# Attention over two heads at once: raw keys and queries are transposed instead of their split parts, in a new order of work

## The chip, the cores and the metric

The kernel runs on one core of a Trainium2 chip. The metric is the device time of one execution in microseconds; of several executions the median counts. The profile is one further execution, recorded by the hardware profiler.

## What is computed

Three stages follow each other. Only the first, attention, is touched by the change.

```python
q_pool = q.reshape(B, H, S // 2, 2, D).mean(axis=3)        # B=4, H=8, S=1152, D=64
scores = scale * np.matmul(q_pool, k.transpose(0, 1, 3, 2)) # 576 x 1152 for each head
scores = scores - np.max(scores, axis=-1, keepdims=True)
attn = np.exp(scores)
attn = attn / (np.sum(attn, axis=-1, keepdims=True) + 1e-09)
return np.matmul(attn, v).astype(np.float32)
# then: mixture of experts on 2304 rows of 512 (top-1 of 8 experts), then a gated two-layer network
```

## The kernel before

Every large product is made nearly exact from rounded parts: a number x is held as hi (x rounded to the matmul's fp32r format) and lo (x - hi). In a score, one operand is 128 rows deep: 64 rows of hi of the keys and 64 rows of lo, against queries of which the part is repeated in both halves. Two matmuls then add up all four products of parts.

Attention goes through 16 pairs of heads. For a pair there are nine query tiles of 128 rows (four of each head, and tile 8, TC, with the 64 rows that are left over of both heads) against 1152 keys, 9 chunks of 128. A tile needs: scores (two halves of 512 keys into the S banks, a ring of three, and a rest of 128 into bank R), the largest of each half (VectorE), exponentials with their sums (ScalarE), transposes of the probabilities (TensorE, f32), a split of these into p_hi (ScalarE) and p_lo (VectorE), and the products with v in bank O.

The work of a pair is written out by hand as a list of units: b0 to b8 (probabilities of the second head of the pair before), c0 to c2 (its tile 8), x (turning the outputs back and dividing), a0 to a8 (the first head of this pair), and g (groups of four chunks of keys and queries of the next pair). TensorE fills a transpose bank T (a ring of three, TR) for each unit; ScalarE and VectorE empty it. The list before, SLOTS, has 33 units in nine slots, one slot a tile; scores, maxima and exponentials of the next tile are put at the first and second place of each slot. The products of a unit come two units after its transposes (LAG = 2), and the rings p_hi and p_lo have PT = 3 buffers.

Keys and queries are prepared thus (split_kq_of, L389 to L399): for each pair, GpSimd adds the two rows of each query pair and writes hi and lo of keys and queries side by side, 36 chunks of 128 columns, in 11.8 us or so of its time; this runs two pairs ahead. TensorE transposes the 36 chunks in nine groups (L697), ScalarE copies each group into kq_t with the scale (L493), and GpSimd pads the rest of the queries with zeros (pad, c_pad). The DMA queue of SyncE (SP) loads keys, queries and values, one DMA for the keys of both heads (rows of 2304 bytes), and waits with next_kq for the split, not for TensorE.

Bodies are unrolled by kind: "first" (pair 0, only a and g units), "mid" (pairs 1 to 14, a loop of two), "last" (pair 15, no g) and "tail".

Of the kernel before, what the change touches and what calls it, by code (L numbers as in the profile page):

```python
# [12 lines left out]
P = 128  # L13
# [48 lines left out]
def attention(nc, q, k, v, w_gate, w_out_gate, w1, x_dram, xs_dram, ys_dram, shared):  # L62
# [15 lines left out]

    B, H, SK, D = k.shape
# [11 lines left out]
    NT = KC + 2 * TILES  # L91
    GROUPS = NT // 4


    HALF_SCALE = (0.5 / float(D) ** 0.5) ** 0.5
    X_TILES = [(0, 3), (3, 6), (6, 8)]
# [3 lines left out]
    PT = 3  # L100


    SCORES_AT, MAXIMA_AT, EXP_AT = (0, 1), (0, 1), (0, 0, 1)
    LAG = 2
    assert (CH, QT, REM, D, PAIRS % 2, NT % 4) == (9, 4, 64, 64, 0, 0)
# [15 lines left out]
    assert all(half.shape[1] == NT * P for half in shared.x_half)  # L121
    assert HALF_SCALE == 0.25 and len([s for slot in SLOTS for s in slot]) % TR == 0 and 2 * TILES % SR == 0
    KEEP = {"first": "ag", "mid": "abcxg", "last": "abcx", "tail": "bcx"}

    def slots(kind):
        return [[s for s in slot if s[0] in KEEP[kind]] for slot in SLOTS]

    def steps(kind):
        return [s for slot in slots(kind) for s in slot]
# [7 lines left out]
    def by_act(step):  # L137

        return step[0] == "g"

    def by_dve(step):
        return not by_act(step)
# [19 lines left out]

    def lagged(kind, j):
# [5 lines left out]
    UNIT_LAST = {"a": ("a", CH - 1), "b": ("b", CH - 1), "c": ("c", 2)}  # L169

    ctx = ExitStack()
    with ctx:
# [12 lines left out]
        q_sum = sb("q_sum", [P, TILES * D])  # L185

        split_kq = [half[:, :].bitcast(F32R) for half in shared.x_half]
        v_hl = [sb(f"v_hl{i}", [P, KC * P], F32R) for i in range(2)]
        kq_t = [sb(f"kq_t{i}", [P, NT * P], F32R) for i in range(2)]
        c_pad = [sb(f"c_pad{i}", [P, 4 * P], F32R) for i in range(2)]  # L190
# [26 lines left out]
        first_q_sums = sem("first_q_sums")  # L217
        first_parts_done = sem("first_parts_done")
        kq_split = sem("kq_split")
        v_split = sem("v_split")  # L220
        c_padded = sem("c_padded")
# [7 lines left out]
        t_free_act = sem("t_free_act")  # L229
        t_free_dve = sem("t_free_dve")  # L230
# [12 lines left out]
        KQ_DMAS, X_DMAS = 5, 3  # L243
# [7 lines left out]
        def split_views(par):  # L251

            kq = split_kq[par]
            return (raw_k[:, :].rearrange("p (c d) -> p c d", d=D),
                    raw_q[:, :].rearrange("p (t r d) -> p t r d", t=TILES, r=2),
                    q_sum[:, :].rearrange("p (t d) -> p t d", d=D),
                    kq[:, 0:KC * P].rearrange("p (c s d) -> p c s d", s=2, d=D),
                    kq[:, KC * P:(KC + TILES) * P].rearrange("p (c s d) -> p c s d", s=2, d=D),
                    kq[:, (KC + TILES) * P:NT * P].rearrange("p (c s d) -> p c s d", s=2, d=D))
# [10 lines left out]
        with nc.Block() as block:  # L270

            @block.sync
            def _(sp):
                def load_kq(p):
                    sp.dma_start(raw_k[:, :].rearrange("p (h c) -> p h c", h=2),
                                 k_rows[bass.ds(2 * p, 2)].rearrange("h p c -> p h c")).then_inc(kq_loaded, 16)
# [13 lines left out]
                def next_kq(p):  # L290

                    sp.wait_ge(kq_split, p)
                    load_kq(p)

                def next_v(p):

                    sp.wait_ge(v_split, p)
                    load_v(p)

                def store(p):  # L300


                    kind = {LAST - 1: "last", LAST: "tail"}.get(p, "mid") if isinstance(p, int) else "mid"
                    sp.wait_ge(t_free_dve, upto(p + 1, kind, by_dve, ("x", 2)))
# [10 lines left out]

                load_kq(0)
                load_v(0)
                next_kq(1)
# [11 lines left out]
                next_v(1)  # L330
                next_kq(2)
                next_kq(3)
                next_v(2)
                with sp.Fori(1, LAST - 2) as p:
                    next_kq(p + 3)
                    next_v(p + 2)
                    store(p - 1)
                next_v(LAST)
# [11 lines left out]
                for p in range(LAST - 3, LAST - 1):  # L350
                    store(p)

                sp.wait_ge(t_filled, before(LAST, "last", every))
# [5 lines left out]
                store(LAST - 1)  # L359
                store(LAST)  # L360

            @block.gpsimd
            def _(pool):
                nc.gpsimd.memset(zeros[:, :], 0.0).then_inc(zeros_ready, 1)
                nc.gpsimd.memset(ident[:, :], 0.0)
                for i in range(2):
                    nc.gpsimd.memset(c_pad[i][:, :].bitcast(F32), 0.0)
# [3 lines left out]
                                        base=0, pattern=[[-1, P]], channel_multiplier=1)  # L371
                nc.gpsimd.affine_select(out=stack2[:, :], in_=stack2[:, :], compare_op=ALU.not_equal, fill=1.0,
                                        base=0, pattern=[[-1, D]], channel_multiplier=1).then_inc(pool_chain, 1)
                pool.wait_ge(pool_chain, 2)
# [10 lines left out]
                def split_kq_of(p, par, chain):  # L385

                    rk, rq, qs, kp, qh, ql = split_views(par)
                    pool.wait_ge(kq_loaded, 16 * KQ_DMAS * (p + 1))
                    nc.gpsimd.tensor_tensor(qs, rq[:, :, 0, :], rq[:, :, 1, :], ALU.add)  # L389
                    first_part(kp[:, :, 0, :], rk).then_inc(pool_chain, 1)  # L390

                    pool.wait_ge(pool_chain, chain + 1)
                    nc.gpsimd.tensor_tensor(kp[:, :, 1, :], rk, kp[:, :, 0, :].bitcast(F32), ALU.subtract)
                    first_part(qh[:, :, 0, :], qs)
                    first_part(qh[:, :, 1, :], qs).then_inc(pool_chain, 1)

                    pool.wait_ge(pool_chain, chain + 2)
                    for s in range(2):
                        last = nc.gpsimd.tensor_tensor(ql[:, :, s, :], qs, qh[:, :, 0, :].bitcast(F32), ALU.subtract)  # L399
                    last.then_inc(kq_split, 1)  # L400
# [12 lines left out]
                def pad(p, par):  # L413

                    for part in range(2):
                        for h in range(2):
                            src = (KC + part * TILES + TC) * P + h * REM
                            dst = (part * 2 + h) * P + h * REM
                            last = first_part(c_pad[par][:, dst:dst + REM], kq_t[par][:, src:src + REM].bitcast(F32))
                    last.then_inc(c_padded, 1)  # L420


                split_v_of(0, 0, 2)

                pool.wait_ge(t_free_act, before(0, "first", by_act))
                pad(0, 0)

                def body(p, par, kind):
                    chain = 3 + 3 * p
                    if kind == "first" or (kind == "mid" and not isinstance(p, int)):  # L430

                        pool.wait_ge(t_filled, before(p, kind, every))
                        split_kq_of(p + 2, par, chain)
                    else:
                        chain -= 2
# [3 lines left out]
                    split_v_of(p + 1, 1 - par, chain + 2)  # L439

                    pool.wait_ge(t_free_act, upto(p, kind, by_act, ("g", 8)))
                    pad(p + 1, 1 - par)
# [5 lines left out]

                p = LAST - 2
                pool.wait_ge(t_filled, before(p, "mid", every))  # L450
                split_kq_of(p + 2, 1, 3 + 3 * p)
                pool.wait_ge(pv_done, upto(p, "mid", is_prob, ("c", 2)))
                split_v_of(p + 1, 0, 5 + 3 * p)
                pool.wait_ge(t_free_act, upto(p, "mid", by_act, ("g", 8)))
                pad(p + 1, 0)
                body(LAST - 1, 0, "mid")

# [32 lines left out]
            def _(act):  # L490
                def group(par, g, bank):

                    nc.scalar.activation(kq_t[par][:, g * 512:g * 512 + 512], T[bank][:, :], ACT.Copy,  # L493
                                         scale=HALF_SCALE).then_inc(t_free_act, 1)
# [1362 lines left out]
```

## Time and profile before

| | us |
|---|---|
| median of 3 runs | 1524.81 |
| lowest, highest | 1521.59, 1526.77 |
| profiled execution, its time | 1529.89 |
| its span, first to last instruction | 1527.9 |
| TensorE busy (matmuls) | 1425.5 (93%) |
| VectorE busy | 854.6 (56%) |
| ScalarE busy | 684.4 (45%) |
| GpSimd busy | 504.6 (33%) |

The span is what the instructions take; the profiled execution's own time is 2 us more. Attention ends at about 657 us of the span. The shares of busy time are over all three stages: in the first one TensorE, VectorE and ScalarE are all far busier than in the others, and the table of 40 slices shows the DMA rate flat at 54 GB/s over most of attention.

### The profile page before, as it was taken

To read this page: it belongs to the slowest core of one execution; us is meant where nothing else is said; L and a number is where in the kernel's file an instruction comes from. 1 tells how busy PE (TensorE), PEld (TensorE's weight loads), DVE (VectorE), ACT (ScalarE), POOL (GpSimd) and SP (SyncE) were. 2 spreads that over 40 slices of the span, in tenths; PEclk is the share of its full clock that TensorE was granted. 3 is DMA by queue.
4 is the path that set the end of the run, shared out by engine and by line. 5 is a ranking of instruction groups with operands and counts; after the bars stand their busy time and mean duration, and the time that the engine had idled before them with its cause. 6 is when DMAs were issued, how large, how long until landed. Compare 5 with 4: busy or idle time off the path is not lost. (4 is left out here: it accounts for less than half of the span.)

```text
span 1527.9 us, 25839 instructions
## 1 busy us (share of the span) xinstructions
PE 1425.5 (93%) x8085; PEld 1236.9 (81%) x8086; DVE 854.6 (56%) x1602; ACT 684.4 (45%) x1635; POOL 504.6 (33%) x340
## 2 busy tenths in 40 slices
PE   4999999999999999983997899998999999999998
PEld 3788888888888888762786787886999999999997
DVE  4788777777777778755443444443643232323222
ACT  4878888888888887751214301101521111111111
POOL 2664444444444432047728802203201010110000
PEclk9999999999999999995998999999999999999999
DMA  7421111111111121245626713112521010100000
GB/s 263 127 56 54 54 54 54 54 54 54 54 54 54 54 65 31 75 139 206 221 96 208 245 41 96 55 41 88 157 65 35 7 35 7 34 7 21 0 21 21
DMA packets 87034, 117.00 MB, mean 77 GB/s; under 512 B 8784, under 2 KB 47696, under 8 KB 86992
## 3 DMA queue, kind: packets, MB, share of 16 engines
q1 hardware_dynamic: 71072, 74.50, 15.6%
q10 hardware_dynamic: 12880, 31.99, 6.2%
q0 software_dynamic: 3040, 9.96, 2.0%
q8 instruction: 25, 0.41, 0.1%
q14 instruction: 17, 0.14, 0.0%
HBM read 87.33 MB, written 29.10 MB: 76 GB/s over the span
## 5 line engine op out<-in xcount | busy, mean ns | idle before, releaser
L648 DVE TENSOR_TENSOR p_lo<-ps_t,p_hi 128x512 fp32r<-128x512 f32 (+1 forms) x336 | 221.3, 670 | 81.7 <-ACT p_hi L509 78.5
L509 ACT ACTIVATE p_hi<-ps_t 128x512 fp32r<-128x512 f32 (+1 forms) x336 | 193.0, 585 | 73.8 <-PE ps_t L697 71.8
L573 DVE TENSOR_REDUCE maxima<-ps_s 128x1 f32<-128x512 f32 x288 | 196.6, 683 | 33.0 <-PE ps_s L804 30.8
L1039 POOL TENSOR_TENSOR w_parts<-raw_w,w_parts 128x1024 fp32r<-128x1024 f32 x64 | 150.9, 2394 | 190.4 <-ACT w_parts L1109 190.2
L533 ACT ACTIVATE probs<-ps_s,neg_max 128x512 f32<-128x512 f32 x288 | 199.9, 694 | 15.7 <-DVE neg_max L586 15.6
L697 PE MATMUL ps_t<-ident,probs 128*128 128x128 f32 x1296 | 191.5, 273 | 0.0
L697 PEld LDWEIGHTS ps_t<-ident,probs 128*128 128x128 f32 x1296 | 156.6, 140 | 33.2
L1655 ACT ACTIVATE silu<-ps_g 128x384 f32<-128x384 f32 x72 | 35.4, 491 | 314.8 <-PE ps_g L1761 314.8
L804 PE MATMUL ps_s<-kq_t 128*128 128x512 f32 x512 | 168.1, 410 | 4.9 <-ACT probs L533 3.1
L1109 ACT ACTIVATE w_parts<-raw_w 128x1024 fp32r<-128x1024 f32 x64 | 67.0, 1057 | 222.0 <-PE ps_h L1436 105.0
L1708 DVE TENSOR_TENSOR silu<-ps_g,silu 128x384 f32<-128x384 f32 x72 | 40.1, 557 | 210.3 <-ACT silu L1655 210.2
L773 PE MATMUL ps_o<-p_hi,v_hl 128*128 128x512 f32 x288 | 138.9, 482 | 12.6 <-DVE p_lo L648 8.1
L804 PEld LDWEIGHTS ps_s<-kq_t 128*128 128x128 f32 x512 | 89.4, 189 | 30.3 <-ACT probs L533 13.5
L773 PE MATMUL ps_o<-p_lo,v_hl 128*128 128x512 f32 x288 | 113.5, 394 | 0.0
L493 ACT ACTIVATE kq_t<-ps_t 128x512 fp32r<-128x512 f32 x144 | 85.0, 604 | 44.9 <-PE ps_t L697 43.8
L1759 PE MATMUL ps_g<-mxt_hi,wg 128*128 128x384 f32 x288 | 97.6, 339 | 2.5 <-DVE mxt_lo L1683 2.4
L1617 POOL DMA_INDIRECT kept_rows<-y_by_slot,slot_i x15 | 15.7, 1048 | 250.2 <-PE ps_turn L1745 235.8
L1761 PE MATMUL ps_g<-mxt_hi,wg 128*128 128x384 f32 x288 | 97.7, 339 | 0.0
L1760 PE MATMUL ps_g<-mxt_lo,wg 128*128 128x384 f32 x288 | 97.3, 338 | 0.0
L1434 PE MATMUL ps_h<-w_parts,xst_hi 128*128 x200 | 83.2, 416 | 14.3 <-POOL w_parts L1039 12.2
L1759 PE MATMUL ps_v<-mxt_hi,wv 128*128 128x384 f32 x288 | 96.4, 335 | 0.0
L1760 PE MATMUL ps_v<-mxt_lo,wv 128*128 128x384 f32 x288 | 96.4, 335 | 0.0
(212 smaller groups left out, 3210.8 us busy)
## 6 DMA issues: line engine op xcount, KB each, us to landing
raw_w<-in_moe_w ACTq DMA_DIRECT2D x61, 512.0 KB, 4.1
raw_k<-in_k SPq DMA_DIRECT2D x16, 576.0 KB, 4.0
raw_v<-in_v SPq DMA_DIRECT2D x16, 576.0 KB, 3.8
raw_q<-in_q SPq DMA_DIRECT2D x32, 256.0 KB, 4.0
x_by_slot<-zeros SPq DMA_DIRECT2D x1, 6400.0 KB, 19.5
y_by_slot<-x_out SPq DMA_DIRECT2D x25, 256.0 KB, 2.0
kept_rows<-x_by_slot SPq DMA_DIRECT2D x23, 256.0 KB, 2.7
out<-kept_rows SPq DMA_DIRECT2D x18, 256.0 KB, 2.2
```

The lines of the kernel that those rows point to most:

```text
L493: nc.scalar.activation(kq_t[par][:, g * 512:g * 512 + 512], T[bank][:, :], ACT.Copy, scale=HALF_SCALE).then_inc(t_free_act, 1)
L509: nc.scalar.activation(p_hi[m % PT][:, 0:w], T[ring(kind, j)][:, 0:w], ACT.Copy).then_inc(hi_ready, 1)
L533: nc.scalar.activation(probs[:, at:at + 512], S[(2 * tile + h) % SR][:, :], ACT.Exp, bias=neg_max[:, tile:tile + 1], accum_out=sums[par][: ...
L573: nc.vector.reduce_max(maxima[:, 3 * tile + h:3 * tile + h + 1], S[(2 * tile + h) % SR][:, :], AX).then_inc(max_done, 1)
L648: nc.vector.tensor_tensor(p_lo[m % PT][:, 0:w], t[:, 0:w], p_hi[m % PT][:, 0:w].bitcast(F32), ALU.subtract).then_inc(t_free_dve, 1)
L697: last = nc.tensor.transpose(dst[:, n * P:(n + 1) * P], src, ident[:, :])
L773: last = nc.tensor.matmul(O[:, :], v_hl[v_par][:, c * P:(c + 1) * P], part[:, :], start=(i == 0 and n == 0), stop=(i == CH - 1 and n == 1))
L804: last = nc.tensor.matmul(S[(2 * tile + h) % SR][:, :], w, kq_t[par][:, at:at + 512], start=(n == 0), stop=(n == len(ops) - 1))
L1039: nc.gpsimd.tensor_tensor(w_part(n, parity, 1, at, PIECE), raw[j % RAW][:, :], w_part(n, parity, 0, at, PIECE).bitcast(F32), ALU.subtract) ...
L1759: nc.tensor.matmul(dst, wh, xh, start=(c == 0), stop=False)
L1760: nc.tensor.matmul(dst, wh, xl, start=False, stop=False)
L1761: last = nc.tensor.matmul(dst, wl, xh, start=False, stop=(c == DC - 1))
```

## The change

Keys and queries are no longer split before they are transposed. The raw keys of the two heads are loaded side by side (chunk, head, 64 columns), the sums of queries likewise, and 14 chunks of 128 columns (9 of keys, 5 of queries) are transposed in four groups. A transposed chunk then holds head 0 in rows 0 to 63 and head 1 in rows 64 to 127. ScalarE writes hi from the bank (group_hi), VectorE writes lo from the bank and hi (group_lo, one or two instructions), both into one tile, parts. Scores need hi and lo of one head below each other, so six DMAs (copy_parts) copy rows of parts into kq_t: for each head 64 rows of 2432 columns (hi of keys, hi and lo of queries), 64 rows of 1152 (lo of keys) and 64 rows of 1280 (queries again).

Also changed: GpSimd only adds queries (q_sums) and splits v; pad and c_pad are gone, since the zeros of q_sum give the padding. The keys come with two DMAs a pair, in runs of 64 numbers. One semaphore t_free takes the place of two. LAG is 3 and PT is 7. The list UNITS has 27 units (four g, two x), and the places of scores, maxima and exponentials are written as the number of a unit for each tile. In the SP queue next_pair waits for the last group of the pair, then issues the six copies, then the loads of the keys and queries after that, then waits for the split of v and loads v. TensorE waits ahead of g0 for the loads and the sums.

```diff
-    NT = KC + 2 * TILES
-    GROUPS = NT // 4
+    QC = QT + 1
+    KQ = CH + QC
+    HEAD = (CH + 2 * QC) * P
+    LO_Q, LO_K = KQ * P, (KQ + QC) * P
+    GROUP_CHUNKS = [(0, 4), (4, 8), (8, 12), (12, 14)]
+    GROUPS = len(GROUP_CHUNKS)
...
-    PT = 3
-    SCORES_AT, MAXIMA_AT, EXP_AT = (0, 1), (0, 1), (0, 0, 1)
-    LAG = 2
-    SLOTS = [
-        [("b", 0), ("g", 0), ("b", 1), ("g", 1)],
-        [("b", 2), ("b", 3), ("b", 4)],
-        [("b", 5), ("b", 6), ("b", 7), ("b", 8), ("g", 2)],
-        [("c", 0), ("c", 1), ("g", 3), ("c", 2), ("g", 4)],
-        [("x", 0), ("a", 0), ("a", 1)],
-        [("x", 1), ("a", 2), ("g", 5), ("g", 6), ("a", 3)],
-        [("a", 4), ("g", 7)],
-        [("g", 8), ("a", 5), ("a", 6)],
-        [("x", 2), ("a", 7), ("a", 8)],
-    ]
+    PT = 7
+    LAG = 3
+    UNITS = [
+        ("g", 0), ("b", 0), ("b", 1), ("b", 2), ("b", 3), ("b", 4), ("b", 5), ("b", 6), ("b", 7),
+        ("b", 8), ("c", 0), ("c", 1), ("c", 2), ("g", 1), ("x", 0), ("a", 0), ("x", 1), ("a", 1),
+        ("a", 2), ("g", 2), ("g", 3), ("a", 3), ("a", 4), ("a", 5), ("a", 6), ("a", 7), ("a", 8),
+    ]
+    SCORES_AT = [(25, 26), (0, 1), (2, 3), (6, 7), (10, 12), (12, 14), (16, 16), (19, 20), (22, 23)]
+    MAXIMA_AT = [(24, 25), (0, 0), (3, 3), (5, 7), (11, 12), (13, 14), (16, 16), (18, 19), (20, 22)]
+    EXP_AT = [(0, 0, 1), (2, 3, 4), (5, 5, 7), (9, 11, 12), (13, 13, 13), (16, 16, 16), (18, 19, 20), (21, 21, 22), (24, 25, 25)]
...
 load_kq(p), SP
-                    sp.dma_start(raw_k[:, :].rearrange("p (h c) -> p h c", h=2),
-                                 k_rows[bass.ds(2 * p, 2)].rearrange("h p c -> p h c")).then_inc(kq_loaded, 16)
+                    for h in range(2):
+                        sp.dma_start(raw_k[:, :].rearrange("p (c h d) -> p c h d", h=2, d=D)[:, :, h, :],
+                                     k_rows[bass.ds(2 * p + h, 1)].rearrange("h p (c d) -> (h p) c d", d=D)
+                                     ).then_inc(kq_loaded, 16)
...
+                def copy_parts(par):
+                    for h in range(2):
+                        src, at = parts[h * D:h * D + D].bitcast(F32), h * HEAD
+                        sp.dma_start(kq_t[par][0:D, at:at + HEAD].bitcast(F32), src[:, 0:LO_K]).then_inc(kq_copied, 16)
+                        sp.dma_start(kq_t[par][D:P, at:at + CH * P].bitcast(F32), src[:, LO_K:LO_K + CH * P]
+                                     ).then_inc(kq_copied, 16)
+                        sp.dma_start(kq_t[par][D:P, at + CH * P:at + HEAD].bitcast(F32), src[:, CH * P:LO_K]
+                                     ).then_inc(kq_copied, 16)
...
+                def next_pair(p, par, kind, load=True):
+                    sp.wait_ge(t_free, upto(p, kind, every, LAST_G))
+                    copy_parts(1 - par)
+                    if load:
+                        load_kq(p + 2)
+                        sp.wait_ge(v_split, p + 2)
+                        load_v(p + 2)
...
+                def q_sums(p):
+                    rq = raw_q[:, :].rearrange("p (t r d) -> p t r d", t=TILES, r=2)
                     pool.wait_ge(kq_loaded, 16 * KQ_DMAS * (p + 1))
+                    for h in range(2):
+                        tiles = slice(h * QT, (h + 1) * QT)
+                        last = nc.gpsimd.tensor_tensor(
+                            q_sum[:, 0:2 * QT * D].rearrange("p (t h d) -> p t h d", h=2, d=D)[:, :, h, :],
+                            rq[:, tiles, 0, :], rq[:, tiles, 1, :], ALU.add)
+                    last.then_inc(q_tiles_summed, 1)
+                    pool.wait_ge(q_tiles_summed, p + 1)
+                    for h in range(2):
+                        rows = slice(h * REM, (h + 1) * REM)
+                        nc.gpsimd.tensor_tensor(q_sum[rows, (2 * QT + h) * D:(2 * QT + h + 1) * D],
+                                                rq[rows, TC, 0, :], rq[rows, TC, 1, :], ALU.add).then_inc(q_summed, 1)
+                        pool.wait_ge(q_summed, 2 * p + h + 1)
...
 body(p, par, kind), GpSimd
+                    split_v_of(p + 1, 1 - par, 3 + p)
+                    if sums:
+                        pool.wait_ge(t_filled, upto(p, kind, every, LAST_G))
+                        q_sums(p + 2)
...
+                def group_lo(g, bank):
+                    c0, c1 = GROUP_CHUNKS[g]
+                    cuts = [c0] + [c for c in (CH,) if c0 < c < c1] + [c1]
+                    for a, b in zip(cuts, cuts[1:]):
+                        at = low_part(a)
+                        last = nc.vector.scalar_tensor_tensor(
+                            out=parts[:, at:at + (b - a) * P], in0=T[bank][:, (a - c0) * P:(b - c0) * P],
+                            scalar=HALF_SCALE, in1=parts[:, a * P:b * P].bitcast(F32), op0=ALU.mult,
+                            op1=ALU.subtract)
+                    last.then_inc(t_free, 1)
...
 fill of a g unit, TensorE
-                        pe.wait_ge(kq_split, p + 2)
-                        last = group(1 - par, i, t)
+                        if i == 0:
+                            pe.wait_ge(kq_loaded, 16 * KQ_DMAS * (p + 2))
+                            pe.wait_ge(q_summed, 2 * (p + 2))
+                        last = group(i, t)
...
 scores(p, par, tile, h), TensorE
-                    if tile == TC and h == 0:
-                        pe.wait_ge(c_padded, p + 1)
+                    if tile == 0 and h == 0:
+                        pe.wait_ge(kq_copied, 16 * COPIES * (p + 1))
```

## Rows read from the trace of the kernel before

**Rows 1.** Busy time by engine in one pair's period: PE, PEld, DVE, ACT, POOL.
```profile
139.40:178.30 38.90, 38.04 (x249) 32.22 (x248) 30.91 (x64) 31.44 (x84) 18.75 (x13) 1.00 0.19 53
```
**Rows 2.** Timeline of GpSimd: start, length, operation; both start a pair's body.
```profile
139.42 1.42 POOL L389 TENSOR_TENSOR q_sum<-raw_q 128x576 f32<-128x576 f32 x1 [5.96 <-PE ps_t L697]
...
489.58 1.43 POOL L389 TENSOR_TENSOR q_sum<-raw_q 128x576 f32<-128x576 f32 x1 [5.96 <-PE ps_t L697]
```
**Rows 3.** Waits in the same period: who, for whom, total, times, longest.
```profile
DVE p_lo L648 <- ACT p_hi L509: 5.2, 10, 1.3
```
**Rows 4.** Timeline of TensorE in that period: starts give the pace.
```profile
163.56 0.62 PE L804 MATMUL ps_s<-kq_t 128*128 128x512 f32 x2
164.02 0.60 PE L697 MATMUL ps_t<-ident,probs 128*128 128x128 f32 x4
164.37 0.48 PE L773 MATMUL ps_o<-p_hi,v_hl 128*128 128x512 f32 x1
...
164.92 0.63 PE L804 MATMUL ps_s<-kq_t 128*128 128x512 f32 x2
165.39 1.03 PE L697 MATMUL ps_t<-ident,kept_rows 128*128 128x128 f32 x8
166.18 0.47 PE L773 MATMUL ps_o<-p_hi,v_hl 128*128 128x512 f32 x1
...
170.75 1.20 PE L804 MATMUL ps_s<-kq_t,c_pad 128*128 128x512 f32 x4
171.78 0.60 PE L697 MATMUL ps_t<-ident,probs 128*128 128x128 f32 x4
...
176.75 1.00 PE L817 MATMUL ps_r<-kq_t 128*128 128x128 f32 x8
177.59 1.06 PE L697 MATMUL ps_t<-ident,probs 128*128 128x128 f32 x8
```
**Rows 5.** Instructions by form in that period, VectorE, then ScalarE.
```profile
L573 DVE TENSOR_REDUCE maxima<-ps_s 128x1 f32<-128x512 f32 x18 | 12.3, 683 | 1.2 <-PE ps_s L804 1.1
L648 DVE TENSOR_TENSOR p_lo<-ps_t,p_hi 128x512 fp32r<-128x512 f32 x18 | 12.2, 690 | 4.0 <-ACT p_hi L509 3.9
L648 DVE TENSOR_TENSOR p_lo<-ps_t,p_hi 128x384 fp32r<-128x384 f32 x3 | 1.7, 555 | 1.3 <-ACT p_hi L509 1.3
...
L493 ACT ACTIVATE kq_t<-ps_t 128x512 fp32r<-128x512 f32 x9 | 5.3, 604 | 2.3 <-PE ps_t L697 2.2
```
**Rows 6.** Timeline of the SP queue: issues of one pair's loads.
```profile
191.01 0.40 SPq L275 DMA_DIRECT2D raw_k<-in_k  x1
191.51 0.42 SPq L279 DMA_DIRECT2D raw_q<-in_q  x1
...
193.47 0.52 SPq L282 DMA_DIRECT2D raw_q<-in_q  x1
```
**Rows 7.** Stretches with transfers: last two columns are DMA share and GB/s.
```profile
24.00:26.00 2.00, 0.68 (x7) 0.53 (x5) 1.95 (x5) 0.00 (x0) 0.00 (x0) 1.00 1.05 408
...
192.00:193.00 1.00, 1.00 (x7) 0.78 (x7) 0.48 (x3) 0.79 (x2) 0.00 (x0) 1.00 0.91 180
...
195.00:196.00 1.00, 1.00 (x10) 1.00 (x10) 1.00 (x2) 0.50 (x1) 0.00 (x0) 1.00 1.12 269
```
**Rows 8.** DMA issues: count, KB each, median us to landing.
```profile
raw_k<-in_k SPq DMA_DIRECT2D x16, 576.0 KB, 4.0
```
**Rows 9.** Timeline of GpSimd: the padding, four instructions of 64 columns.
```profile
171.26 1.15 POOL L383 TENSOR_TENSOR c_pad<-kq_t,zeros 128x64 fp32r<-128x64 f32 x4 [5.62 <-ACT kq_t L493]
```
**Rows 10.** Timeline of TensorE at the start: first scores, first g of body 0.
```profile
22.64 1.19 PE L804 MATMUL ps_s<-kq_t 128*128 128x512 f32 x4 [0.81 <-ACT kq_t L493]
...
29.16 1.09 PE L697 MATMUL ps_t<-ident,x_half 128*128 128x128 f32 x4 [4.48 <-DVE x_half L683]
```
**Rows 11.** Stretches at the start: third column from the end is PEclk.
```profile
26.00:28.00 2.00, 0.00 (x0) 0.00 (x0) 1.94 (x3) 1.26 (x2) 0.00 (x0) 0.65 1.04 406
28.00:30.00 2.00, 0.84 (x5) 0.87 (x5) 1.01 (x2) 0.00 (x0) 0.00 (x0) 0.50 1.05 408
```

More of the change, by code:

```diff
@@ L169, in attention @@
     UNIT_LAST = {"a": ("a", CH - 1), "b": ("b", CH - 1), "c": ("c", 2)}
+    LAST_X = ("x", len(X_TILES) - 1)
+    LAST_G = ("g", GROUPS - 1)
+    assert sum(map(is_prob, UNITS)) % PT == 0 and LAG < PT
+    assert UNITS[-LAG:] == [("a", CH - LAG + j) for j in range(LAG)]
     ctx = ExitStack()
@@ L184, in attention @@
         raw_q = sb("raw_q", [P, TILES * 2 * D])
[L185 to L187 removed]
+        q_sum = sb("q_sum", [P, 2 * QC * D])
+        parts = shared.x_half[0][:, 0:LO_K + CH * P].bitcast(F32R)
         v_hl = [sb(f"v_hl{i}", [P, KC * P], F32R) for i in range(2)]
[L189 to L190 removed]
+        kq_t = [sb(f"kq_t{i}", [P, 2 * HEAD], F32R) for i in range(2)]
         probs = sb("probs", [P, TILES * SK])
@@ L411, in split_v_of, with body @@
                                             ).then_inc(v_split, 1)
[L413 to L420, printed above, removed]
-                split_v_of(0, 0, 2)
[L425 to L435, printed above, removed]
+                q_sums(0)
+                split_v_of(0, 0, 2)
+                pool.wait_ge(t_filled, GROUPS)
+                q_sums(1)
+                def body(p, par, kind, sums=True):
                     if kind != "first":
                         pool.wait_ge(pv_done, upto(p, kind, is_prob, ("c", 2)))
-                    split_v_of(p + 1, 1 - par, chain + 2)
-                    pool.wait_ge(t_free_act, upto(p, kind, by_act, ("g", 8)))
-                    pad(p + 1, 1 - par)
+                    split_v_of(p + 1, 1 - par, 3 + p)
+                    if sums:
+                        pool.wait_ge(t_filled, upto(p, kind, every, LAST_G))
+                        q_sums(p + 2)
                 body(0, 0, "first")
@@ L447, in _ @@
                     body(p + 1, 0, "mid")
[L449 to L456, printed above, removed]
+                body(LAST - 2, 1, "mid")
+                body(LAST - 1, 0, "mid", sums=False)
                 nc.gpsimd.memset(shared.ones[:, :], 1.0)
@@ L686, in _ @@
-                second_parts(0)
+                    for n, step in enumerate(UNITS):
+                        if step in steps(kind):
+                            take(p, par, kind, j, step)
+                            if lagged(kind, j) in UNIT_LAST.values():
+                                outputs(p, kind, lagged(kind, j)[0])
+                            j += 1
+                        for tile in (*range(1, TILES), 0):
+                            if kind == "tail" or (kind == "last" and tile == 0):
+                                continue
+                            of = p if tile else p + 1
+                            if MAXIMA_AT[tile][0] == n:
+                                largest_half(of, tile, 0)
+                            if MAXIMA_AT[tile][1] == n:
+                                largest_half(of, tile, 1)
+                                largest_rest(of, tile)
@@ L687, in _ @@
+                    if kind == "tail":
+                        for n in range(j, j + LAG):
+                            if lagged(kind, n) in UNIT_LAST.values():
+                                outputs(p, kind, lagged(kind, n)[0])
+                for g in range(GROUPS):
+                    dve.wait_ge(kq_hi_done, g + 1)
+                    group_lo(g, g % TR)
                 largest_half(0, 0, 0)
@@ L806, in scores, with scores_rem @@
                     last.then_inc(s_ready, 1)
-                def scores_rem(p, par, tile, waits=True):
-                    if waits:
+                def scores_rem(p, par, tile, opening=False):
+                    if not (opening and tile == 0):
                         pe.wait_ge(exp_rem_done, TILES * p + tile)
@@ L847, in _ @@
-                pe.wait_ge(consts_ready, 1)
-                pe.wait_ge(kq_split, 1)
+                    for n, step in enumerate(UNITS):
+                        if step in steps(kind):
+                            fill(p, par, kind, j, step)
+                            done = lagged(kind, j)
+                            if done is not None and is_prob(done):
+                                products(p, par, kind, j - LAG, done)
+                            j += 1
+                        for tile in (*range(1, TILES), 0):
+                            if kind == "tail" or (kind == "last" and tile == 0):
+                                continue
+                            of = (p, par) if tile else (p + 1, 1 - par)
+                            opening = kind == "first" and tile > 0
+                            if SCORES_AT[tile][0] == n:
+                                scores(*of, tile, 0, opening)
+                            if SCORES_AT[tile][1] == n:
+                                scores(*of, tile, 1, opening)
+                                if tile % QT == 0:
+                                    scores_rem(*of, tile, opening)
@@ L849, in _ @@
+                    if kind == "tail":
+                        for n in range(j, j + LAG):
+                            if is_prob(lagged(kind, n)):
+                                products(p, par, kind, n - LAG, lagged(kind, n))
+                pe.wait_ge(consts_ready, 2)
+                pe.wait_ge(kq_loaded, 16 * KQ_DMAS)
+                pe.wait_ge(q_summed, 2)
                 for g in range(GROUPS):
                     if g >= TR:
-                        pe.wait_ge(t_free_act, g - TR + 1)
@@ L853, in _ @@
-                    group(0, g, T[g % TR]).then_inc(t_filled, 1)
-                pe.wait_ge(t_free_act, before(0, "first", by_act))
-                scores(0, 0, 0, 0, waits=False)
-                scores(0, 0, 0, 1, waits=False)
-                scores_rem(0, 0, 0, waits=False)
+                        pe.wait_ge(t_free, g - TR + 1)
+                    group(g, T[g % TR]).then_inc(t_filled, 1)
+                scores(0, 0, 0, 0, True)
+                scores(0, 0, 0, 1, True)
+                scores_rem(0, 0, 0, True)
```

262 lines of the change are left out of this document (88 added, 174 removed).

## The prediction

> **What bounds the kernel now.** I read the table of 40 slices first (attention is the first 17), then the busy time of one period, the waits in it, the timelines, and last the DMA views. A pair's body takes (489.58 - 139.42) / 9 = 38.9 us [rows 2]. In it TensorE is busy for 38.0 us, VectorE 30.9, ScalarE 31.4, GpSimd 18.8, the DMA engines 19% [rows 1]. So TensorE is the bound of attention, and VectorE and ScalarE have 8 us each to spare. VectorE waits 5.2 us for ScalarE's p_hi [rows 3], which costs nothing while TensorE is full. Nothing waits for a transfer in a period: loads are issued two pairs ahead. Here the reader should see that the change touches not only TensorE's sum but this distance.
>
> **The parts that save.** TensorE: eight transposes take 166.18 - 165.39 = 0.79 us [rows 4], 0.10 each; 22 fewer (36 to 14) save 2.2 us a pair. With one x unit fewer and its last 0.9 us of idle time partly gone, TensorE's own period would be about 36.0 us. ScalarE loses nine copies of 0.60 us and gains three of that and a half one [rows 5]: 31.4 - 3.3 = 28.1. VectorE gains five instructions. The nearest row for 512 columns is p_lo at 0.69 us and for 384 at 0.555 [rows 5]; by these 0.69 + 0.69 + (0.28 + 0.56) + 0.42 = 2.6 us, so 33.5. If the new form cost as little as a maximum (0.68) nothing changes; at twice its price VectorE would be at 36 and equal to TensorE. GpSimd loses over 10 us of 18.8, all of it hidden already. LAG 3 and PT 7 take waits of TensorE for p_lo away, at most the 0.9 us above; the ring T of three still makes a fill wait for the unit three back. If nothing else happened, a period would be 36 to 37.5 us.
>
> **The chain that is added.** Raw keys, q_sum and parts exist once. TensorE may turn g0 of a body only when the loads for it have landed, and SP issues these only after VectorE's lo of g3 in the body before and after the six copies. g3 is unit 20 of 27, g0 is unit 0. So each period holds, one after the other: the work from g0 to the lo of g3 (call it W), and the chain from there back to the next g0 (call it C). The period is W + C if that is over 38.9.
>
> C, step by step. SP wakes and issues: 0.2. From an issue to the first bytes 1.0: the load issued at 191.01 [rows 6] shows no share before 192, then 0.91 [rows 7]. The copies: 2 heads x 64 rows x 4864 columns x 4 bytes = 2.49 MB. No row shows a copy from SBUF to SBUF, nor one whose ends are 64 partitions. Ends: 408 GB/s, the fastest stretch, a write of long rows from all partitions, gives 6.1 us; the slowest stretch with busy engines, 180 GB/s at a share of 0.91, so 198, gives 12.6 us [rows 7]. Every fast row has all 128 partitions at its SBUF end, and here both ends have half of them, so I take the slow end, 12.6, and keep both for the range. Then the loads, behind the copies in the same queue: keys and queries 1.18 MB in short packets, 269 GB/s [rows 7], 4.4 us (3.3 at the best neighbouring rate, 6.0 at 198). To the receipt 1.3 (an issue lands in 4.0 [rows 8], of which 1.0 is the start and about 1.6 the bytes of 576 KB). GpSimd's q_sums: 1.42 us for 576 columns [rows 2], so 0.63 for each of two of 256, and two of 64 columns at 0.3 [rows 9], with handshakes 2.2, and 0.2 for TensorE to wake: 2.4. C = 0.2 + 1.0 + 12.6 + 4.4 + 1.3 + 2.4 = 21.9 us. SP's twelve issues, about 0.6 apart [rows 6], take 7 us and lie beside the transfers.
>
> The Trainium skill has a rule that speaks against this change ("SBUF — State Buffer", section "Door 1: The DMA port swizzle (why `[64,N]` ≈ `[32,N]`)"): partitions 0 to 63 reach half of the DMA ports, so a transfer to 64 partitions is no faster than one to 32; it gives about 196 to 218 GB/s. By it the copies would take 11.4 to 12.7 us. No run here shows it yet.
>
> W, step by step. TensorE's work after the fill of g3 up to the next g0: five products at 0.55 (the two g units have none), six fills at 0.35 to 0.40, scores of tile 7's second half 0.46, of tile 8 2 x 1.03 and its rest 0.4, of tile 0 2 x 0.46 and its rests 0.84 [rows 4]: 9.7 to 10 us. TensorE needs 35.4 us a pair without idle time, so 25.3 from g0 to the fill of g3, and 1.3 more until VectorE has emptied it. VectorE's own work in that stretch: 12 b and c units 7.9, three a units 2.1, maxima of seven tiles 14 x 0.683 + 1.8, outputs, normalisers and x units 3.9, groups 2.6: 27.9 as a sum of durations, 25.3 at the ratio of union to sum of rows 1 and its forms (30.9 to 34.1). It starts with an empty pipeline: ScalarE must copy g0 before the exponential of tile 0, on which tile 1's second half waits; that is 2.5 us. W = 28 (26.5 to 29).
>
> Period = 28 + 21.9 = 49.9 us, 11.0 more than before.
>
> **The sum.** From body 1 to body 15 there are 14 periods: 154 us. The start: before, the first scores are at 22.6 and g0 of body 0 at 29.2 [rows 10]; body 1 starts at 139.42 - 2 x 38.9 = 61.6. After, loads land at 7.3 and sums at 9.5, four groups are empty at about 14, so g0 of body 0 is at 14 + 21.9 = 36, its g3 at about 58 (body 0 has only the 13 a and g units and is bound by exponentials) and g0 of body 1 at 80: 18 us later. Body 15 has no g0 and waits for the copies alone: 4 us less. 154 + 18 - 4 = 168. The profiled execution's own 1529.9 + 168 = 1698; its median of runs is 5 lower: 1693. The later stages are the same instructions; the loads of x wait for copies that are long done.
>
> What I leave out and keep in the range: TensorE stops twice a period, for the copies ahead of tile 0's scores and again ahead of g0, some 10 us in all. After 4.5 us of idle [rows 10] the granted clock is 0.65, then 0.50, that is 1.2 instead of 2.4 GHz [rows 11].
>
> **The rivals.**
> Copies at full rate: 6.1 us as by the 408 GB/s row. C = 15.4, period 43.4, 14 x 4.5 = 63, start 6, end -2: +67, 1592. For it: the engines hold that rate for 15 us at the start. Against it: half of the partitions at both ends.
> The clock too: in each period TensorE works for 3 us or more at half speed after the stops and that lies in W. +3 a pair over the forecast: 1735. For it: rows 11. Against it: the stop is in two parts, with 3 us of scores between, and VectorE sets much of W.
> The chain is hidden, and the change is faster: the DMA engines pass over the copies and serve the loads beside them, and TensorE runs ahead enough. It decides where W + C is below 38.9, with C below 10.9 at W = 28. Then the period is TensorE's and VectorE's 36 to 36.5: 15 x -2.5 = -38, 1487. Against it: with transfers that take no time, the last of twelve issues still starts at 6.6, lands 4.0 later and the sums take 2.4: C = 13.2. That would give 41 us, and 1560.
> VectorE as the bound at twice the price for the lo parts would add 2.6 to W, as part of the forecast's own range.
>
> **How the numbers follow.** Forecast (slow copies, clock little) 0.55, its own range 1660 to 1725; full-rate copies 0.27; clock too 0.12; hidden 0.06. Within the cases: faster by over 0.3% has 0.05, within 0.3% 0.01, slower 0.94; 0.3% (5 us) is about what a measurement of this kernel can tell from none. The range 1585 to 1750 holds the full-rate case, the forecast and the clock case, and leaves out the hidden one and the tails.
>
> **What would show it.** After: the period 50 us (43 to 52), with TensorE waiting ahead of L804 of tile 0 for copies into kq_t, and ahead of a transposing group for GpSimd's q_sum or the loads, 8 us or more in sum a pair; kq_t copies landing 12 to 14 us after their first issue; transposes of keys and queries 14 a pair; VectorE busy 33 to 34 us a period; DMA share up to about 0.6 of the period. It would be wrong if the copies land within 8 us, or if no wait stands ahead of g0; the step at fault would then be the copies' rate or the order of the queue.

## The result: 13% slower, and where the time went

The changed kernel takes 1722.31 us in the median of 4 runs (1717.25 to 1724.0), the kernel before 1525.79 (1521.59 to 1527.8). The ratio is 1.129, with a 95% interval of 1.125 to 1.132. 1693 was forecast, in a range of 1585 to 1750. The profiled execution has a span of 1720.3 us, 192.4 more than before.

One period of a pair, by engine (columns as in [rows 1]), then the starts of GpSimd's split of v, which comes once a body; the first of these is body 1, the last body 14:

```profile
321.10:372.20 51.10, 38.37 (x226) 32.36 (x225) 32.66 (x67) 28.89 (x80) 7.35 (x6) 0.87 0.41 89
```
```profile
111.09 2.66 POOL L397 TENSOR_TENSOR v_hl<-raw_v,zeros 128x1152 fp32r<-128x1152 f32 x1 [23.95 <-PE ps_o L762]
...
774.05 2.66 POOL L397 TENSOR_TENSOR v_hl<-raw_v,zeros 128x1152 fp32r<-128x1152 f32 x1 [22.75 <-issue]
```

The period is (774.05 - 111.09) / 13 = 51.0 us, where it was 38.9 [rows 2]; from one g0 to the next it is 51.1. TensorE's busy time has hardly changed (38.4, was 38.0 [rows 1]), though it has 22 transposes fewer: it works part of the time at half its clock (0.87 in the mean). VectorE has 32.7 instead of 30.9, ScalarE 28.9 instead of 31.4, GpSimd 7.4 instead of 18.8. The period has grown by 12 us in which TensorE stands still. The timeline of TensorE has both stops; the rows are the last g group of one pair, the first scores of the next pair, its g0, and its last g group:

```profile
318.10 0.44 PE L686 MATMUL ps_t<-ident,q_sum 128*128 128x128 f32 x2 [0.31 <-DVE p_lo L649]
...
335.19 1.19 PE L784 MATMUL ps_s<-kq_t 128*128 128x512 f32 x2 [9.86 <-DMA kq_t<-kept_rows]
...
342.32 1.12 PE L686 MATMUL ps_t<-ident,raw_k 128*128 128x128 f32 x4 [2.49 <-POOL q_sum L413]
...
369.26 0.44 PE L686 MATMUL ps_t<-ident,q_sum 128*128 128x128 f32 x2 [0.31 <-DVE p_lo L649]
```

The reader should see 9.86 us of idle time whose releaser is a copy into kq_t (the profile calls the tile parts "kept_rows"), and 2.49 us whose releaser is GpSimd's sum of queries. Neither releaser is in the waits of before. The queue of SP shows the beginning of the chain, and GpSimd's timeline its end:

```profile
321.09 0.49 SPq L295 DMA_DIRECT2D kq_t<-kept_rows  x1
321.62 0.60 SPq L296 DMA_DIRECT2D kq_t<-kept_rows  x1
322.26 2.39 SPq L298 DMA_DIRECT2D kq_t<-kept_rows  x1
...
330.61 3.46 SPq L275 DMA_DIRECT2D raw_k<-in_k  x2
...
372.25 0.50 SPq L295 DMA_DIRECT2D kq_t<-kept_rows  x1
```
```profile
340.07 1.41 POOL L405 TENSOR_TENSOR q_sum<-raw_q 128x256 f32<-128x256 f32 x2 [20.79 <-DMA raw_q<-in_q]
341.56 0.71 POOL L413 TENSOR_TENSOR q_sum<-raw_q 64x64 f32<-64x64 f32 x2
```

So C, from the first copy's issue to g0, is 342.32 - 321.09 = 21.2 us, and W, from g0 to the next first issue, 372.25 - 342.32 = 29.9. They add up to the period.

### The profile page after: what moved, and what is told of

It is laid out like the page before. It is cut to its first block and busy times, and to the rows that moved or that the text cites. A ratio compares the mean times of both kernels' runs of the same rounds, so it can differ in the third digit from the quotient of the medians.

```text
span 1720.3 us, 24853 instructions
## 1 busy us (share of the span) xinstructions
PE 1433.4 (83%) x7733; PEld 1236.4 (72%) x7734; DVE 871.5 (51%) x1658; ACT 639.0 (37%) x1549; POOL 345.1 (20%) x241
## 5 line engine op out<-in xcount | busy, mean ns | idle before, releaser
L784 PE MATMUL ps_s<-kq_t 128*128 128x512 f32 x640 | 228.7, 455 | 171.0 <-DMA kq_t<-kept_rows 163.9
L784 PEld LDWEIGHTS ps_s<-kq_t 128*128 128x128 f32 x640 | 124.9, 214 | 207.5 <-issue 154.4
L649 DVE TENSOR_TENSOR p_lo<-ps_t,p_hi 128x512 fp32r<-128x512 f32 (+1 forms) x336 | 215.0, 666 | 14.0 <-ACT p_hi L506 9.3
L686 PE MATMUL ps_t<-ident,probs 128*128 128x128 f32 x1296 | 207.5, 286 | 0.0
L686 PEld LDWEIGHTS ps_t<-ident,probs 128*128 128x128 f32 x1296 | 171.8, 149 | 46.6 <-issue 6.3
L753 PE MATMUL ps_o<-p_hi,v_hl 128*128 128x512 f32 x288 | 148.1, 514 | 1.9 <-DVE o_sb L590 1.9
L753 PE MATMUL ps_o<-p_lo,v_hl 128*128 128x512 f32 x288 | 121.0, 420 | 0.0
L397 POOL TENSOR_TENSOR v_hl<-raw_v,zeros 128x1152 fp32r<-128x1152 f32 x16 | 42.4, 2651 | 318.8 <-PE ps_o L762 295.6
L1738 PE MATMUL ps_v<-mxt_hi,wv 128*128 128x384 f32 x288 | 96.4, 335 | 0.0
L1740 PE MATMUL ps_v<-mxt_hi,wv 128*128 128x384 f32 x288 | 96.4, 335 | 0.0
```

The costliest lines, as they stand in the source:

```text
L649: nc.vector.tensor_tensor(p_lo[n][:, 0:w], t[:, 0:w], p_hi[n][:, 0:w].bitcast(F32), ALU.subtract).then_inc(t_free, 1)
L686: last = nc.tensor.transpose(dst[:, n * P:(n + 1) * P], src, ident[:, :])
L753: last = nc.tensor.matmul(O[:, :], v_hl[v_par][:, c * P:(c + 1) * P], part[:, :], start=(i == 0 and n == 0), stop=(i == CH - 1 and n == 1))
L784: last = nc.tensor.matmul(S[(2 * tile + h) % SR][:, :], w, kq_t[par][:, at:at + 512], start=(n == 0), stop=(n == len(ops) - 1))
L1738: nc.tensor.matmul(dst, wh, xh, start=(c == 0), stop=False)
L1740: last = nc.tensor.matmul(dst, wl, xh, start=False, stop=(c == DC - 1))
```

## The experiments

The ratios are against the kernel before on the same chip; chips differ by up to 0.3%, so a difference of a few us between two rows is read from their ratios. The periods are means over bodies 3 to 14, from the starts of GpSimd's split of v; the first bodies are still settling and are left out. The kernels down to LAG 2 are edits of the changed kernel; those with early groups build on one another; the last is an edit of the kernel before.

| kernel | median us | ratio, 95% interval | period us |
|---|---|---|---|
| changed kernel | 1722.31 | 1.129, 1.125 to 1.132 | 51.1 |
| copies over 128 partitions | 1639.35 | 1.075, 1.072 to 1.077 | 46.0 |
| short copies | 1622.22 | 1.062, 1.060 to 1.065 | 44.3 |
| loads ahead of copies | 1741.09 | 1.140, 1.138 to 1.142 | 52.8 |
| TensorE warm in the first stop | 1726.76 | 1.129, 1.126 to 1.132 | 51.1 |
| warm in both stops | 1703.65 | 1.115, 1.112 to 1.117 | 49.5 |
| LAG 2 | 1767.29 | 1.158, 1.155 to 1.162 | 54.2 |
| early groups | 1548.61 | 1.014, 1.012 to 1.016 | 39.1 |
| early groups, LAG 2 | 1592.16 | 1.041, 1.039 to 1.043 | 42.0 |
| early groups, zeros later | 1547.43 | 1.011, 1.009 to 1.014 | 39.1 |
| the same, x later | 1554.59 | 1.015, 1.013 to 1.017 | 39.7 |
| the same, O copied by ScalarE | 1515.82 | 0.991, 0.989 to 0.994 | 37.2 |
| kernel before, LAG 3 | 1560.04 | 1.020, 1.017 to 1.022 | 40.7 |

**Are the copies slow because of their 64 partitions?**

```diff
-                        src, at = parts[h * D:h * D + D].bitcast(F32), h * HEAD
-                        (three DMAs of 64 rows: HEAD, CH * P and HEAD - CH * P columns)
+                        at, src = h * HEAD, parts[:, :].bitcast(F32)
+                        for w0, w1 in ((0, 1216), (1216, 1792), (1792, 2432)):
+                            sp.dma_start(kq_t[par][:, at + w0:at + w1].bitcast(F32), src[:, w0:w1]
+                                         ).then_inc(kq_copied, 16)
```

> The six copies of a pair move the same 2.49 MB in six DMAs of the same bytes, but over all 128 partitions at both ends (half as many columns each). kq_t then holds the wrong rows. Theory (the copies are slow because each end reaches only half of the partitions): the copies take 6 to 7 us instead of 13, the stop ahead of tile 0's scores shrinks from 9.9 to about 3 us, the period falls from 51.1 to about 44, the kernel to about 1610 us. Rival (a copy from SBUF to SBUF runs at about 190 GB/s whatever its rows): nothing moves, 1722.

The copies now take about 6.5 us of transfer, from 338 to 344.4, and the wait for them falls to 4.47. First two stretches of the changed kernel while it copies, then two of this one (last columns: clock, DMA share, GB/s), then this one's stop:

```profile
326.00:327.00 1.00, 0.00 (x0) 0.00 (x0) 0.00 (x0) 0.97 (x4) 0.00 (x0) 1.00 1.02 214
...
332.00:333.00 1.00, 0.00 (x0) 0.00 (x0) 0.00 (x0) 0.00 (x0) 0.00 (x0) 0.50 1.04 219
```
```profile
340.00:341.00 1.00, 1.00 (x9) 0.81 (x7) 0.96 (x4) 0.87 (x2) 0.00 (x0) 1.00 1.03 397
341.00:342.00 1.00, 0.39 (x2) 0.00 (x0) 0.93 (x2) 1.00 (x4) 0.00 (x0) 1.00 1.05 421
```
```profile
345.85 1.19 PE L782 MATMUL ps_s<-kq_t 128*128 128x512 f32 x2 [4.47 <-DMA kq_t<-kept_rows]
```

At the same share of the DMA engines, the same bytes move at twice the rate. That settles the copies' price: the number of partitions, not the SBUF to SBUF path. (The edit also keeps each row at its own partition, where four of the six copies of the changed kernel move rows across to the other 64. That isn't what cost: by the bytes moved until then, the stretch from 326 lies in such copies and the one from 332 in those that keep their rows in place, and their rates are 214 and 219 GB/s.) It is also what the Trainium skill says ("SBUF — State Buffer", section "Door 1: The DMA port swizzle (why `[64,N]` ≈ `[32,N]`)"): by that rule 64 partitions move at about half; here it was 2.49 MB in 13 us (322 to 335), 192 GB/s, so the trace agrees. The bytes took 6.5 us less, but C fell only by 5.3, to 15.9 us (353.04 - 337.12), as the loads behind the copies took 6.2 us to their landing instead of 5.0. W is 29.7 and 30.7 us in turn, and the period 45.6 and 46.6, 46.0 in the mean. The expectation of 44 missed that.

**What is left without the bytes of the copies?**

```diff
-                    copy_parts(1 - par)
+                    copy_parts(1 - par, full=kind == "first")
+ (each copy of the later pairs: a, b, c = (P, P, P) columns)
```

> From the third pair on, each of the six copies moves only 128 columns (0.2 MB in all), so kq_t keeps old values elsewhere; waits and issues stay. Theory (the period is W + C, and C has the copies' bytes in it): C falls from 21.2 to about 13, bound by twelve issues, a landing and the sums; the period falls to 40 to 41 us, the kernel to about 1570. Rival (VectorE or the new order of work is what lengthens the period): it stays at 46 us or more, 1650 or above.

C is 353.59 - 339.94 = 13.7 us, near the 13.2 that the prediction had as its floor. But the period is 44.3, not 40 to 41: neither theory's number. W is 384.35 - 353.59 = 30.8 us, 0.9 more than in the changed kernel. What lengthened it is the clock: TensorE still stops for 5.62 us ahead of g0, and works at half its clock for 5 us after it, where it was 3.3 us in the changed kernel:

```profile
353.59 1.11 PE L687 MATMUL ps_t<-ident,raw_k 128*128 128x128 f32 x4 [5.62 <-POOL q_sum L414]
```
```profile
353.00:356.00 3.00, 2.41 (x8) 2.12 (x9) 0.55 (x1) 1.18 (x4) 0.46 (x2) 0.50 0.19 55
356.00:359.00 3.00, 3.00 (x11) 2.30 (x11) 0.83 (x2) 1.70 (x6) 0.00 (x0) 0.53 0.00 0
```

**Is the queue served in order?**

```diff
-                    copy_parts(1 - par)
                     if load:
                         load_kq(p + 2)
+                    copy_parts(1 - par)
```

> SP issues the loads of keys and queries ahead of the six copies. Theory (one queue, served in order, and both waits count): the loads land within 7 us and g0 no longer waits for them, but the copies land at about 19 instead of 14 us, and g0 stands behind the scores of tile 0 that wait for them; C becomes 23 to 24, the period 53 to 54, the kernel 1750 to 1760. Rival (only the loads, which come last, count, since the copies could have been hidden): the period falls to 47, the kernel to 1665.

The period is 53.2 and 52.2 in turn, 52.8 in the mean, where the theory had 53 to 54; the kernel, at 1741, is somewhat better than its 1750. The stop ahead of the scores is 15.36 us now, and there is none ahead of g0:

```profile
345.64 1.19 PE L784 MATMUL ps_s<-kq_t 128*128 128x512 f32 x2 [15.36 <-DMA kq_t<-kept_rows]
350.79 0.81 PE L686 MATMUL ps_t<-ident,raw_k 128*128 128x128 f32 x4
```

So what stands first in the queue lands first, and both of its parts are on the chain. The rival in which the loads pass by the copies falls.

**What does the clock cost?** Two kernels, the second with both edits (neither for the first pair):

```diff
 scores(...), ahead of the wait for kq_copied
+                            for n in range(85):
+                                nc.tensor.transpose(S[(2 * tile + h) % SR][:, 0:P], ident[:, :], ident[:, :])
 fill(...), ahead of the wait for kq_loaded at g0
+                                for n in range(32):
+                                    nc.tensor.transpose(t[:, 0:P], ident[:, :], ident[:, :])
```

> The changed kernel, and TensorE transposes the identity 85 times (about 9 us) into the S bank that it is about to fill, ahead of each pair's wait for the copies; nothing else moves. Theory (the stops cost more than their own length, since TensorE then works at 0.5 of its clock in W): the granted clock stays at 1.00, the work from g0 to g3 falls by 1.5 to 2.3 us, the period from 51.1 to 49 to 49.6, the kernel to about 1697. Rival (VectorE sets W, the clock costs nothing): 1722 as before, or more.

Missed: 1726.76, period 51.1. The first stop was filled, but the second grew to 4.27 us, as the scores in front of it were done sooner, and the clock fell there instead. The stretch at g0 of this kernel, then one of the kernel with both stops filled:

```profile
344.00:346.00 2.00, 1.93 (x7) 1.74 (x8) 0.07 (x1) 0.70 (x2) 0.01 (x1) 0.52 0.12 34
```
```profile
337.00:341.00 4.00, 4.00 (x24) 3.27 (x24) 2.40 (x5) 3.37 (x10) 0.00 (x0) 1.00 0.05 13
```

> As the kernel that transposes the identity 85 times ahead of the wait for the copies, and 32 times more (3.4 us) ahead of the wait of g0, into the T bank that g0 fills. In the run before this one the clock held 1.00 through the first stop and fell after the second, and the period did not move. Theory (the clock that falls after the second stop is what lengthens W): the granted clock is 1.00 at g0, the period falls from 51.1 to 49 to 49.8, the kernel to about 1700. Rival (VectorE sets W): 1722 or more.

1703.65 us, period 49.5, as expected. From g0 to the last group TensorE now takes 25.4 us instead of 26.9:

```profile
336.86 0.66 PE L686 MATMUL ps_t<-ident,raw_k 128*128 128x128 f32 x4 [0.76 <-POOL q_sum L413]
...
362.21 0.44 PE L686 MATMUL ps_t<-ident,q_sum 128*128 128x128 f32 x2 [0.31 <-DVE p_lo L649]
```

The clock thus costs 1.6 us a pair, beside the stops themselves: 19 us in the medians, 23 against the kernel before on each one's chip. Over the kernels, TensorE takes 25.4 us from g0 to the last group with no stretch at half clock behind g0, 26.9 with 3.3 us of it, and 27.8 with 5 us.

**Is it where the groups stand?** Only the list changes:

```diff
-        ("g", 0), ("b", 0), ("b", 1), ("b", 2), ("b", 3), ("b", 4), ("b", 5), ("b", 6), ("b", 7),
-        ("b", 8), ("c", 0), ("c", 1), ("c", 2), ("g", 1), ("x", 0), ("a", 0), ("x", 1), ("a", 1),
-        ("a", 2), ("g", 2), ("g", 3), ("a", 3), ("a", 4), ("a", 5), ("a", 6), ("a", 7), ("a", 8),
+        ("b", 0), ("b", 1), ("b", 2), ("b", 3), ("g", 0), ("b", 4), ("b", 5), ("g", 1), ("b", 6),
+        ("b", 7), ("g", 2), ("b", 8), ("g", 3), ("c", 0), ("c", 1), ("c", 2), ("x", 0), ("a", 0),
+        ("x", 1), ("a", 1), ("a", 2), ("a", 3), ("a", 4), ("a", 5), ("a", 6), ("a", 7), ("a", 8),
```

> Only UNITS changes: the four groups stand at units 4, 7, 10 and 12 instead of 0, 13, 19 and 20, so 12 units lie between g3 and the scores that need the copies, and 18 between g3 and the next g0. Theory (the loss is the chain from g3 to the next g0, not the work): the chain of 21 us lies beside other work, TensorE is full again, the period is 36.5 to 38 us, the kernel 1490 to 1515. Rival (copies or VectorE's added work cost wherever they stand): the period stays above 40, the kernel above 1550.

174 us of the 196 lost come back, with every copy and every load still there. This is the main evidence that the chain's place, not its work, is the cause. But the period is 39.1, a little over the kernel before, where 36.5 to 38 was expected. TensorE is busy for 35.8 us of a period in the mean of two, 2.3 less than before, and waits for the rest. Two waits a pair stand out, both for VectorE's copies of O:

```profile
PE ps_t L717 <- DVE o_sb L593: 23.8, 15, 2.4
...
PE ps_o L753 <- DVE o_sb L590: 14.9, 15, 1.1
```

The rest of its 22 us over the kernel before is the start: the split of v in body 1 begins at 101.6 instead of 82.3, 19 us later. Of these, 6.7 are the first scores, at 29.3 instead of 22.6 [rows 10], since they need the first copies. What the other 12 are made of isn't shown; the granted clock was 0.66 to 0.80 from 30 to 60 us there, where it was 0.83 to 1.00 before, and a stop of 4.3 us for copies stands at 69 us.

**What is LAG 3 worth?** In the kernel with early groups, LAG = 3 becomes 2.

> The kernel with the early groups, with products two units back (LAG 2) instead of three. Theory (the ring T of three already makes a fill wait for the unit three back, so LAG 3 gains little once the chain is hidden): TensorE waits for p_lo some 1 us a pair more, 1552 to 1565 instead of 1549. Rival (LAG 3 delays the copies of O, for which x units and the first products of b wait, and so costs): 1535 to 1545.

1592.16: 43 us slower, and both theories missed its size. The period is 42.0, 3.0 us longer. The waits for p_lo ahead of products come back (L753, 1.6 us in one period), the one for a copy of O ahead of b's first product grows from 1.0 to 1.8, and one of 0.7 for VectorE's reading of c's outputs out of O is new; that of 1.5 at x0 is gone. Then the same edit in the changed kernel itself:

> The changed kernel with products two units back instead of three; the one line changes. Theory (in this order of units LAG 3 is worth 3 us a pair, and some three quarters of a pair's units lie in W, outside the chain of transfers): W grows by 2 to 2.5 us, the period to 53.1 to 53.6, the kernel to about 1752. Rival (the stops for the transfers give VectorE time to catch up, so that the lag costs nothing): 1722.

1767.29, the period 54.2, 3 us longer and not 2 to 2.5: the stops for the transfers hide nothing of it. And the other way, in the kernel before (LAG 3, PT 7 with prob_ring, a6 moved behind x2):

> The kernel before the change, with products three units back and seven buffers of p_hi and p_lo, and a6 moved one place, behind x2. Theory (in that kernel TensorE is full: 0.9 us of idle time a pair is all that LAG 3 can give): period 38.0 to 38.9, 1512 to 1526. Rival (products three back delay the copies of O and so cost): 1530 to 1545.

1560.04, 2.0% slower than with LAG 2, the period 40.7. The rival holds in sign and goes beyond its size: between 140 and 640 us, TensorE's waits for the copy of O grow from 1.0 to 15.2 us in all, as the rival has it, and those for ScalarE's exponentials, of which it says nothing, from 0.5 to 17.1. The same lag helped in one order of units and came with a loss in the other. Which of the three edits costs here wasn't separated.

**Three more steps on the early groups.** next_pair(0, 0, "first") ahead of the two DMAs of zeros:

> The kernel with the early groups, and the two DMAs that write 8.2 MB of zeros are issued after the second pair's copies and loads instead of ahead of them. Theory (most of what is left of the loss is the start, where those zeros stand in the queue ahead of the copies of pair 1): the stop of 4.3 us at 69 us and part of the late first bodies go, 1537 to 1543 instead of 1549. Rival (the start is bound by the first copies and the exponentials alone): 1549.

1547.43: no difference from 1548.61 that can be told. The rival holds: the zeros weren't what delays the start. Then x0 and x1 one unit later:

> As the kernel with the zeros later, and the two x units stand one unit later, at 17 and 19, behind a0 and a1. Theory (TensorE waits 1.5 us in each pair at x0 for the copy of O by VectorE): that wait goes, the period falls by 1 to 1.5 us, 1520 to 1530, level with the kernel before. Rival (without x0 between them the first product of a waits for the copy of c's outputs instead): 1537 to 1550.

1554.59: the rival holds. The wait moved from x0 to the first products of c and a. Then, on the kernel with the zeros later, the copies of O by ScalarE:

```diff
-                        nc.vector.tensor_copy(o_sb[:, 0:512], O[:, :]).then_inc(o_free, 1)
...
+                            if done == UNIT_LAST["a"]:
+                                act.wait_ge(pv_done, before(p, kind, is_prob))
+                                nc.scalar.activation(o_sb[:, 0:512], O[:, :], ACT.Copy).then_inc(o_free, 1)
+ (the same for unit b)
```

> The kernel with early groups and later zeros, with the copies of O after the units a and b (one 128x512 copy each) made by ScalarE instead of VectorE. Theory (with the chain hidden, what eats TensorE's saving of 2.6 us are waits for VectorE, 2.5 us of them for these two copies): TensorE's waits at x0 and at the first product of b shrink, the period goes from 39.0 to about 37.5, 1525 to 1532. Rival (ScalarE in its place waits for the products itself and delays p_hi): 1545 or above.

1515.82 us, 0.9% faster than the kernel before (0.989 to 0.994) and below the 1525 to 1532 expected; the period is 37.2. Its busy time and its largest wait of TensorE for a copy of O:

```profile
325.00:362.50 37.50, 36.09 (x231) 30.28 (x230) 32.63 (x67) 29.85 (x83) 8.17 (x7) 1.00 0.57 126
```
```profile
PE ps_t L718 <- ACT o_sb L545: 0.8, 1, 0.8
```

This is the version that beats both, with the transposes of the change, its groups early and its VectorE relieved.

## Why the prediction was right, point by point

The direction, the cause and the mechanism are those of the prediction: the period is W + C, TensorE stops twice, and the chain runs from VectorE's lo of g3 over copies, loads and sums to g0. The time, 1722, lies 29 us above the point forecast and in the upper part of its range. By terms:

- **C**, forecast 21.9 with wake-ups of 0.2 at its head and its end, measured 21.2 from the first issue. No row stands behind the 0.2; the last sum ends at 342.27 and g0 starts at 342.32. The copies' transfer was 13 us (forecast 12.6); the 6.1 of the full-rate rival was measured only with 128 partitions. The loads behind them, in packets down to 256 bytes, took 5.0 us with the landing (335.1 to 340.07), forecast 5.7 (4.4 + 1.3); q_sums ran 2.2 us, as forecast.
- **W**, forecast 28, measured 29.9. TensorE from g0 to the fill of g3: forecast 25.3, measured 26.9, and 25.4 with the clock held up. The clock's rival was therefore true, but at half its size: 1.6 us a pair and not 3. The kernel that kept TensorE busy in both stops shows it. From that fill to the first issue: forecast 1.3, measured 372.25 - 369.26 = 3.0, because VectorE has two maxima and the lo of g2 to do first. W = 28 was taken from VectorE, 25.3 us of its work and 2.5 for the start with an empty pipeline. VectorE does work for 25.2 us in W, but it doesn't set it: with the clock held up, W fell to 28.3 and VectorE's work stayed at 25.1. The 2.5 aren't needed, so 28 was the right size with the wrong parts, and that it came out near is luck. This is the step that failed in its reasons.
- **VectorE's lo parts**: forecast 0.69 for 512 columns; the row below has 0.692. Its busy time is 32.7 in 51 us, near the 33.5 forecast.

```profile
L561 DVE SCALAR_TENSOR_TENSOR kept_rows<-ps_t,kept_rows 128x512 fp32r<-128x512 f32 x2 | 1.4, 692 | 2.8 <-ACT kept_rows L487 2.8
```

- **The sum**: 192.4 us of span = start 25.6 + 14 x 12.2 - 4. Forecast was 18 + 14 x 11.0 - 4 = 168. The start is the difference of body 1's beginning (its g0 at 87.2, was 61.6). The -4 is what is left over, and that it equals the forecast's is partly luck: attention alone ends at 852.2 us instead of 656.9, 195.3 later, and the later stages take 2.9 us less in this execution, so the last body gives only 1. The forecast for g0 of body 0 (36) held, at 37.6. Body 0 itself was mis-sized: its first copy is issued at 65.9 and not at 58. That is 8 us of the 24 that were missing, the period's 1.2 us the other 17. TensorE's granted clock was 0.50 from 30 to 60 us (0.83 to 1.00 before), which the forecast of the start leaves out; what it costs there wasn't measured.
- **The signs**: the two waits (12.4 us a pair), the landing of the copies (14 us after the first issue) and VectorE's busy time are as named; the DMA share of a period is 0.41, where up to 0.6 was named.
- **LAG 3**, forecast as worth at most the 0.9 us of idle time, since a fill waits for the unit three back anyway. This was wrong: in the changed order it is worth 3 us a pair, and without it the kernel is 45 us slower. It was read from the kernel before, in which products were rarely late.
- **The engine-bound period** was forecast at 36 to 37.5 for a hidden chain. With the chain hidden it was 39.1, and 37.2 only with the copies of O moved. TensorE's saving of 2.2 us is real (busy 35.8), but it went into waits for VectorE. The hidden rival's 1487 us would not have been reached by hiding the chain alone.

## What to carry to other kernels

Where a change replaces buffers that are filled ahead by single ones, find the last instruction that frees each and the first that needs it again, and add up all that stands between, the queue's earlier transfers too: here 21 us of transfers and sums lay in a gap of six units, from g3 to the next g0, where the early groups leave 18 of the same 27. Moving the groups in the list gave back 174 of 196 us; making the copies twice as fast gave 83. And when the bounding engine gets less work, look next at who empties its last bank: here the gain came only when that work was moved to the engine with time to spare.

## What the runs showed of the hardware

- Copies between rows of 64 partitions ran at 192 GB/s with a DMA share of 1.0, the same bytes over 128 partitions at 380 to 420.
- An issue on SP took 0.5 us with an empty queue and 2.4 us behind two other copies. With copies of 128 columns all six issues took 0.5 to 0.6 us, so SP, too, is held by long transfers.
- Keeping TensorE busy through one stop of 10 us gained nothing, because a second stop of 4.3 us right behind it brought the granted clock to 0.5 as well. Only both together gave the 1.6 us. After a stop of 5.6 us ahead of g0 the clock stayed at 0.5 for 5 us of full work.
